# The first two attention units side by side, the second in lent buffers

## The reference

```python
def _attn_ref(q, k, v, alpha):              # (4, 8, 768, 48)
    for t in range(S):
        state = alpha[:, :, t, :, None] * state + einsum('bhd,bhe->bhde', k[:, :, t], v[:, :, t])
        y[:, :, t] = einsum('bhd,bhde->bhe', q[:, :, t], state)

def _moe_ref(x, domain_probs, w1, w2):      # x (3072, 384), 4 experts of 1024
    p = domain_probs / (domain_probs.sum(-1, keepdims=True) + 1e-09)
    for e in range(E):
        out += p[:, e:e + 1] * (maximum(x @ w1[e], 0.0) @ w2[e])

def _moe2_ref(x, w_in, w_out):              # 384 -> 2048 -> 384
    h = x @ w_in
    return (h - tanh(h)) @ w_out
```

## Time and profile before

| what | us |
|---|---|
| median of 3 runs | 1432.39 (1431.64 to 1432.49) |
| the profiled execution, its own time | 1432.69 |
| span of its records | 1430.4 |
| first matmul of unit 0 / of unit 1 / of the dense work | 14.35 / 51.39 / 101.30 |
| PE busy | 1353.6 (95% of the span) |
| DVE / ACT / POOL busy | 864.1 / 559.9 / 296.9 |
| mean granted clock of TensorE | 0.977 of full speed |

### The profile page before, as it was taken

How to read it: one execution, slowest core, us unless ns; L and a number is a source line. 1 busy time by engine, 2 the same in 40 slices (tenths; PEclk the granted TensorE clock), 3 DMA queues, 4 the chain that set the end, 5 groups by cost and what they waited for, 6 DMA issues and landing times.

```text
span 1430.4 us, 25628 instructions
## 1 busy us (share of the span) xinstructions
PE 1353.6 (95%) x10177; PEld 1134.4 (79%) x10177; DVE 864.1 (60%) x1660; ACT 559.9 (39%) x1004; POOL 296.9 (21%) x292
## 2 busy tenths in 40 slices
PE   3438999999999999999999999999999999999999
PEld 2436878898888898787888787889887889888888
DVE  7647484698464487455487546478646458433386
ACT  1222424683223474221375131376131356311175
POOL 5555665400403000312200131300131000000000
PEclk9669999999999999999999999999999999999999
DMA  6228769686655664655565655565555465555552
GB/s 179 73 85 303 263 232 332 234 310 219 218 193 192 223 214 166 220 198 190 195 235 187 208 193 195 185 240 193 191 204 186 155 214 197 187 210 198 177 199 88
DMA packets 104965, 289.05 MB, mean 202 GB/s; under 512 B 10032, under 2 KB 64912, under 8 KB 104848
## 3 DMA queue, kind: packets, MB, share of 16 engines
q1 hardware_dynamic: 104848, 287.43, 58.6%
HBM read 242.52 MB, written 42.52 MB: 199 GB/s over the span
## 4 chain that ended last, share of the span: by engine, by line
PE 87%; DVE 7%; issue 3%; ACT 1%; DMA 0%; SPq 0%; POOL 0%; DVEq 0%; ACTq 0%
PE bank L567 14%; PE bank L568 13%; PE bank L569 13%; PE bank L590 9%; PE bank L591 9%; PE bank L592 9%; PE bank L615 4%; PE bank L613 4%; PE bank L614 4%; PE bank L488 4%; PE bank L523 2%; PE bank L510 1%; DVE R L867 1%; PE bank L466 1%; PE bank L499 1%
## 5 line engine op out<-in xcount | busy, mean ns | idle before, releaser
L743 ACT ACTIVATE HH<-GG 128x512 fp32r<-128x512 f32 x192 | 121.2, 631 | 666.6 <-PE bank L592 532.4
L567 PE MATMUL bank<-XB,RG 128*128 128x512 f32 x864 | 350.3, 405 | 7.1 <-DMA XB<-XS 6.8
L568 PE MATMUL bank<-XB,RG 128*128 128x512 f32 x864 | 340.6, 394 | 0.0
L569 PE MATMUL bank<-XB,RG 128*128 128x512 f32 x864 | 339.6, 393 | 0.0
L941 DVE SCALAR_TENSOR_TENSOR GG<-bank,PB 128x512 f32<-128x512 f32 x192 | 133.2, 694 | 337.6 <-PE bank L569 337.4
L590 PE MATMUL bank<-HH,RG 128*128 128x512 f32 x576 | 224.7, 390 | 1.5 <-ACT OUT L776 1.5
L1080 POOL TENSOR_TENSOR KU<-KU,TOT 128x256 f32<-128x256 f32 x96 | 75.5, 814 | 717.3 <-PE bank L488 717.3
L591 PE MATMUL bank<-HH,RG 128*128 128x512 f32 x576 | 224.3, 389 | 0.0
L592 PE MATMUL bank<-HL,RG 128*128 128x512 f32 x576 | 224.2, 389 | 0.0
L567 PEld LDWEIGHTS bank<-XB,RG 128*128 128x128 f32 x864 | 163.0, 189 | 48.1 <-issue 7.1
L569 PEld LDWEIGHTS bank<-XB,RG 128*128 128x128 f32 x864 | 163.0, 189 | 35.8
(11 more groups left out here) (77 smaller groups left out, 1672.8 us busy)
## 6 DMA issues: line engine op xcount, KB each, us to landing
RG<-scratch SPq DMA_DIRECT2D x240, 768.0 KB, 4.3
scratch<-RG SPq DMA_DIRECT2D x48, 768.0 KB, 5.2
VS<-vp SPq DMA_DIRECT2D x12, 768.0 KB, 6.1
AU<-qka SPq DMA_DIRECT2D x12, 512.0 KB, 5.3
R<-qka SPq DMA_DIRECT2D x12, 512.0 KB, 5.3
KU<-qka SPq DMA_DIRECT2D x12, 512.0 KB, 5.9
WS<-w SPq DMA_DIRECT2D x32, 192.0 KB, 3.0
PB<-probs SPq DMA_DIRECT2D x6, 1024.0 KB, 7.4
```

The source lines that it names most:

```text
L567: nc.tensor.matmul(out, w1(g, 0, kt), x_part(m, 0, kt), start=(kt == 0), stop=False)
L568: nc.tensor.matmul(out, w1(g, 0, kt), x_part(m, 1, kt), start=False, stop=False)
L569: last = nc.tensor.matmul(out, w1(g, 1, kt), x_part(m, 0, kt), start=False, stop=(kt == KT - 1))
```

## The change

Unit 1 gets tiles of its own, which lie over tiles of the dense layers that nothing uses before the dense work (`lend`: KU over SQ, AU over TH, R0, R1 and R2 over HH, HL and GG, SC over QD, QB over LG, KJ and the tables over XB1, VS over OUT), and semaphores of its own. All later units use the old tiles; unit 2 follows unit 0 in them. Units 0 and 1 have four banks each. For every engine the order of the two units' steps is written out. The decay tables of unit 0 and the spreading of the first two units' queries go from POOL to DVE, which starts with them; the probabilities go to the middle of DVE's order, their transpose behind both units' `turn`. POOL makes unit 1's tables between its key steps, waits for `rotated[1]` before it splits the first four weight slots, and then prepares unit 2. `attend` makes the half with the features that have to be moved first, `high_x` and `low_x` copy those first, and `move` starts its first two DMAs when they are there. `join` no longer begins with the copy that needs the last `rotate`. Left out below are the renamed semaphores and tiles of functions that are otherwise the same, and `stated`, `faded` and `carried` counted by set.

```diff
-RING_ALONE = 6
+RING_ALONE = 4
...
+def own(u):
+
+    return int(u == 1)
...
+        def lend(name, words, owner, room, skip=0):
+
+            assert skip + words <= room, name
+            return nc.alloc_sbuf_tensor_at(name, [P, words], fp32, offset=offset[owner] + 4 * skip)
...
+        KU = [place("KU", UW), lend("KUb", UW, "SQ", 2 * TB)]
+        AU = [place("AU", UW), lend("AUb", UW, "TH", 2 * TB)]
+        R0 = [place("R0", QL), lend("R0b", QL, "HH", 4 * TB)]
+        R1 = [place("R1", QL), lend("R1b", QL, "HL", 4 * TB)]
+        R2 = [place("R2", QL), lend("R2b", QL, "GG", 4 * TB)]
+        SC = [place("SC", UW), lend("SCb", UW, "QD", 2 * TB)]
+        QB = [place("QB", UW), lend("QBb", UW, "LG", 2 * TB)]
+        KJ = [place("KJ", UW), lend("KJb", UW, "XB1", 2 * KT * TB)]
+        VS = [place("VS", CHUNKS * VW), lend("VSb", CHUNKS * VW, "OUT", TT * DM)]
...
+        TOT = [place("TOT", TOTALS), lend("TOTb", TOTALS, "XB1", 2 * KT * TB, UW)]
...
-            n = u * FILLS + k
-            return bank[2 + n % RING_ALONE] if u < AHEAD else a_bank[n % 2]
+            return bank[RING_ALONE * u + k % RING_ALONE] if u < AHEAD else a_bank[k % 2]
...
             def move(u):
-                sp.wait_ge(x_low, 3 * u + 3)
-                for hh in range(2):
-                    for j in range(KT):
+                for j in (2, 0, 1):
+                    sp.wait_ge(x_low[own(u)], 3 * turn_of(u) + (2 if j == 2 else 3))
+                    for hh in range(2):
                         src = XS[CH * hh + SPARE * j:CH * hh + SPARE * (j + 1), :].rearrange("p (h t) -> p h t", h=2)
                         dst = x_tile(u)[CH * hh + D:CH * hh + CH, :, j, x_tokens(u)]
-                        sp.dma_start(dst.bitcast(fp32), src.bitcast(fp32)).then_inc(moved, 16)
+                        sp.dma_start(dst.bitcast(fp32), src.bitcast(fp32)).then_inc(moved[own(u)], 16)
...
+            for u in range(AHEAD):
+                load(AU[u][:, :], u, 2, a_in[u])
+                load(R1[u][:, 0:UW], u, 0, q_in[u])
+                load(KU[u][:, :], u, 1, k_in[u])
+                if u == 0:
+                    sp.dma_start(masks[:, :], mask_d).then_inc(masks_in, 16)
+            sp.dma_start(ident[:, :], ident_d).then_inc(ident_in, 16)
+            sp.dma_start(prob[:, :], dp_d).then_inc(prob_in, 16)
+            for u in range(AHEAD):
+                load_values(u)
             for g in range(STAGES):
                 stage(g)
-            for t in range(STAGGER + STEPS):
-                if t < STEPS:
-                    attention(0, t)
-                if t >= STAGGER:
-                    attention(1, t - STAGGER)
-                if t == 2:
-                    sp.wait_ge(prob_laid, 1)
-                    sp.dma_start(probs_d, PT[0:E * NTB * TT, :]).then_inc(prob_saved, 16)
-                    sp.wait_ge(prob_saved, 16)
-                    probs(0)
+            attention(0, 4)
+            attention(0, 7)
+            attention(0, 11)
+            sp.wait_ge(prob_laid, 1)
+            sp.dma_start(probs_d, PT[0:E * NTB * TT, :]).then_inc(prob_saved, 16)
+            sp.wait_ge(prob_saved, 16)
+            probs(0)
+            attention(0, 15)
+            move(0)
+            move(1)
...
-                    c = n * 2 * UC + m
+                    c = (1 - n) * 2 * UC + m
...
-            pe.wait_ge(const_in, 48)
+            diagonal(0)
+            scores(0, 0, 0)
+            diagonal(1)
+            scores(0, 0, 1)
+            scores(1, 0, 0)
+            scores(0, 1, 0)
+            scores(1, 0, 1)
+            scores(0, 1, 1)
+            scores(0, 2, 0)
+            scores(0, 2, 1)
+            scores(1, 1, 0)
+            turn(0, 0)
+            turn(0, 1)
+            scores(1, 1, 1)
+            deltas(0, 0)
+            deltas(0, 1)
+            scores(1, 2, 0)
+            scores(1, 2, 1)
+            turn(1, 0)
+            turn(1, 1)
             pe.wait_ge(prob_step, E + 2)
-            nc.tensor.transpose(h_bank[0][0:E * NTB * TT, 0:P], prob[:, :], ident[:, :]).then_inc(prob_turned, 1)
-            for t in range(STAGGER + STEPS):
-                if t < STEPS:
-                    attention(0, t)
-                if t >= STAGGER:
-                    attention(1, t - STAGGER)
+            nc.tensor.transpose(bank[3][0:E * NTB * TT, 0:P], prob[:, :], ident[:, :]).then_inc(prob_turned, 1)
+            attend(0, 0)
             pe.wait_ge(prob_laid, 1)
+            attend(0, 1)
+            deltas(1, 0)
+            deltas(1, 1)
+            attend(1, 0)
+            attend(1, 1)
...
-                nc.scalar.activation(x[:, 0, 0:2, t], fill_bank(u, 18)[:, :].rearrange("p (a t) -> p a t", a=2),
-                                     ACT.Copy).then_inc(x_high, 1)
-                act.wait_ge(filled, filled_at(u, 19))
-                nc.scalar.activation(x[:, 0, 2, t], fill_bank(u, 19)[:, 0:UT], ACT.Copy).then_inc(x_high, 1)
+                act.wait_ge(filled[own(u)], filled_at(u, 18))
                 if u:
-                    act.wait_ge(moved, 96 * u)
-                nc.scalar.activation(XS[:, 0:UT], fill_bank(u, 19)[:, UT:2 * UT], ACT.Copy).then_inc(x_high, 1)
+                    act.wait_ge(moved[own(u - 1)], 96 * turn_of(u - 1) + 96)
+                nc.scalar.activation(XS[:, 0:UT], fill_bank(u, 18)[:, UT:2 * UT], ACT.Copy).then_inc(x_high[own(u)], 1)
+                nc.scalar.activation(x[:, 0, 2, t], fill_bank(u, 18)[:, 0:UT], ACT.Copy).then_inc(x_high[own(u)], 1)
+                act.wait_ge(filled[own(u)], filled_at(u, 19))
+                nc.scalar.activation(x[:, 0, 0:2, t], fill_bank(u, 19)[:, :].rearrange("p (a t) -> p a t", a=2),
+                                     ACT.Copy).then_inc(x_high[own(u)], 1)
...
-            split = 0
-            for t in range(STAGGER + STEPS):
-                if t < STEPS:
-                    attention(0, t)
-                if t >= STAGGER:
-                    attention(1, t - STAGGER)
-                if t == 0:
-                    act.wait_ge(prob_turned, 1)
-                    nc.scalar.activation(PT[0:E * NTB * TT, :], h_bank[0][0:E * NTB * TT, 0:P],
-                                         ACT.Copy).then_inc(prob_laid, 1)
-                if t in (3, 4, 5, 6):
-                    split_high(t - 3)
+            for g in range(LEAD):
+                split_high(g)
+            lay(0, 0)
+            lay(0, 1)
+            join(0)
+            act.wait_ge(prob_turned, 1)
+            nc.scalar.activation(PT[0:E * NTB * TT, :], bank[3][0:E * NTB * TT, 0:P], ACT.Copy).then_inc(prob_laid, 1)
+            carry(0)
+            lay(1, 0)
+            lay(1, 1)
+            join(1)
+            high_x(0)
+            carry(1)
+            high_x(1)
...
             def low_x(u):
                 x, t = x_tile(u), x_tokens(u)
-                dve.wait_ge(x_high, 3 * u + 1)
-                nc.vector.tensor_tensor(x[:, 1, 0:2, t], fill_bank(u, 18)[:, :].rearrange("p (a t) -> p a t", a=2),
-                                        x[:, 0, 0:2, t].bitcast(fp32), ALU.subtract).then_inc(x_low, 1)
-                dve.wait_ge(x_high, 3 * u + 3)
-                nc.vector.tensor_tensor(x[:, 1, 2, t], fill_bank(u, 19)[:, 0:UT], x[:, 0, 2, t].bitcast(fp32),
-                                        ALU.subtract).then_inc(x_low, 1)
-                nc.vector.tensor_tensor(XS[:, UT:2 * UT], fill_bank(u, 19)[:, UT:2 * UT], XS[:, 0:UT].bitcast(fp32),
-                                        ALU.subtract).then_inc(x_low, 1)
+                dve.wait_ge(x_high[own(u)], 3 * turn_of(u) + 2)
+                nc.vector.tensor_tensor(XS[:, UT:2 * UT], fill_bank(u, 18)[:, UT:2 * UT], XS[:, 0:UT].bitcast(fp32),
+                                        ALU.subtract).then_inc(x_low[own(u)], 1)
+                nc.vector.tensor_tensor(x[:, 1, 2, t], fill_bank(u, 18)[:, 0:UT], x[:, 0, 2, t].bitcast(fp32),
+                                        ALU.subtract).then_inc(x_low[own(u)], 1)
+                dve.wait_ge(x_high[own(u)], 3 * turn_of(u) + 3)
+                nc.vector.tensor_tensor(x[:, 1, 0:2, t], fill_bank(u, 19)[:, :].rearrange("p (a t) -> p a t", a=2),
+                                        x[:, 0, 0:2, t].bitcast(fp32), ALU.subtract).then_inc(x_low[own(u)], 1)
...
+            def tabulate(u, first=0, last=9):
+                n = 9 * turn_of(u)
+                for i in range(first, last):
+                    t, two, three = tables(u, i // 3)
+                    if i:
+                        dve.wait_ge(tabled[own(u)], n + i)
+                    if i % 3 == 0:
+                        out, a, b = two, t[:, :, 0:3], t[:, :, 1:4]
+                    elif i % 3 == 1:
+                        out, a, b = three, two[:, :, 0:2], t[:, :, 2:4]
+                    else:
+                        out, a, b = total(u, i // 3 + 1).rearrange("p (n a) -> p n a", a=1), three[:, :, 0:1], t[:, :, 3:4]
```

(137 more changed lines are left out.)

394 lines of the change are left out of this document (168 added, 226 removed).

## The result

| | before | after |
|---|---|---|
| median | 1432.02 us (4 runs) | 1415.3 us (4 runs, 1413.88 to 1416.52) |
| profiled execution | 1432.69 us, span 1430.4 | 1413.88 us, span 1412.0 |
| first dense matmul | 101.30 | 84.59 |
| from there to the end of the span | 1329.1 | 1327.4 |

The ratio is 0.9881, 95% interval 0.9869 to 0.9894: 1.2% faster, 16.7 us by the medians where 10.2 were forecast. The profiled execution is the fastest of the four, so its 18.4 us of span overstate the typical gain a little.

The account below looks back on a forecast made before the run. PE bounds the dense work, so only its start counts, set by DVE work and hand-overs: 5.5 + 45.2 + 14.4 = 65.1 for the last pick, tail to 91.1, 10.2 us earlier than 101.3; 1432.39 - 10.2 = 1422.2 us, range 1411 to 1428.5.

Parts of the forecast that it names:

- The dense work untouched: After the first dense matmul: the change touches none of these matmuls; only their start moves, 10.2 us earlier.
- half the waits: Case in the front with half of DVE's waits gone: dense start near 82.5, time 1413.5 us.
- Turns: DVE and POOL instructions on SBUF exclude each other: 18 DVE waits, 13.7 us, before unit 1's last pick.
- 45.2 of work: DVE's summed work up to unit 1's last pick, tables through probabilities, at prices from the profile, without waits.
- The walk: Both engines' orders stepped in time with turns on SBUF: last pick at 65.1, dense start at 91.1, ±3.
- The tail: From pick(1,2,0) at 62.6 through attend(0), states(1) to 78.3 and both units' moves: dense start at 91.1.
- The rest: Dense start to end of span: lasts as before, 1329.1 us, ±2.5.
- No turns, or half: Rival in the front: without turns dense start 73.9, 1405.0 us; half 82.5, 1413.5; chance 0.14 for a start before 85.
- The hand-over eats the gain: Rival in the tail: one XS makes the units run one after the other; start 101 to 103, about 1432; chance 0.06.
- Unfair turns: Rival in the front: DVE waits for two POOL instructions each time; doubled, start 111, 1442 us; chance 0.04.
- The clock: Rival at the dense start: clock loss after PE's longer idle doubles, adding 5.5 us, 1428; chance 0.08.
- PE's two waits for join and lay: Before the change, two pieces called "issue", 6.84 and 11.29 us, in which PE waits for ACT.

Follow-up runs that it names:

- its variant: Kernel before with only POOL's four weight splits moved from step 10 of unit 1 to behind prepare(2); 1427.56 us, ratio 0.9965.
- units in turn: Changed kernel with only the order put back: each engine does all of unit 0, then all of unit 1; 1419.97 us, ratio 0.9911.
- tables on POOL: Changed kernel with unit 0's nine tables back on POOL instead of DVE; 1415.63 us.
- two XS: Changed kernel with a second XS tile for unit 1, lent by weight slot RG7, so high_x(1) need not wait for move(0); 1412.82 us.
- transpose early: Changed kernel with the probabilities' transpose ahead of turn(1) in PE's order instead of behind it; 1412.72 us.
- the last kernel: Changed kernel with two XS, POOL held until states(1) ends, transpose early, unit 1's moves on two queues, and the longer hold; 1406.53 us, ratio 0.982.
- the fifth split held: Changed kernel in which POOL waits for unit 2's first rotate before splitting the fifth weight slot; 1414.79 us.
- the longer hold: Changed kernel with POOL's fifth weight split held until queries_up[0] reaches 3 (unit 2's level-1 queries complete); 1415.98 us.

## Why the prediction held, point by point

- *The dense work untouched, the gain all in front of it.* Right: 16.7 of the span's 18.4 us are the earlier start.
- *The number.* In range, but with luck. The start was forecast at 91.1, between 86 and 96 with a chance of 0.68, and came at 84.59. The forecast's own range of time began at 1417; 1415.3 is inside the stated one only because that had been reached down to half the waits, for safety. Of the 6.5 us by which the start was forecast too late, some 5.5 are turns, net of errors of price, and 0.9 is DVE's start (5.5 taken, 4.62 measured).
- *Turns.* Right as a mechanism, by the ends of the instructions in the kernel before. Mis-sized as a term: this is the step behind most of the error. I had 18 waits of 13.7 us before the last pick. DVE is busy from 4.62 to 58.70, 54.1 us; less my own 45.2 of work and 0.7 of gaps, 8.2 are left for turns and errors of price. One such error goes the other way: unit 0's nine tables, priced 2.9, took 4.0 with POOL idle. The walk put keys(1,1) beside rotate(1,1), 5.0 us with 2.1 of waits; in the trace POOL was waiting for PE then, and the rotate took 2.27. It put 1.5 into the tables, where POOL had not yet got its decays, and 0.6 into states(0); both had none. Rotate(0,1) and spread_distant(1), 3.9 of work and 5.7 of waits by the walk, took 7.8. Against that, distant of unit 0 and rotate(0,2) met turns that I did not have, 1.3 and 0.9.
- *The tail.* Every link came as laid out: attend(0) behind turn(1), the transpose, PT and carry(0), 61.25 (66.8 taken); states(1) to 70.9 (78.3), first issue 71.6 (79.1), high_x(1) at the landing of move(0), 77.85 (84.3), PE's pause 9.8 us (9.5). Two errors partly cancel in it: from attend(0) to the end of states(1) 9.7 us for 11.5 taken, and from the first issue to the dense start 13.0 us for 12.0, where one of the issues took 1.41 us in place of 0.63.
- *The rest.* Taken as equal, measured 1.7 us shorter. The stretch of 30 us from the dense start, in the trace of before and of after:

```profile
101.30:131.30 30.00, 26.19 (x264) 20.20 (x264) 22.97 (x43) 7.43 (x12) 12.45 (x8) 0.83 0.82 282
```

```profile
84.59:114.59 30.00, 26.18 (x269) 20.24 (x270) 24.18 (x44) 8.20 (x12) 12.89 (x9) 0.88 0.85 285
```

 Columns: stretch, length, busy us of PE, weight loads, DVE, ACT and POOL, then the granted clock, the share of the DMA engines and GB/s. PE is busy as long, at a clock of 0.88 instead of 0.83, so more is done. The difference lies behind PE's pause of 3.8 us: over the 5 us from 15 us after the dense start on, the clock is 0.77 instead of 0.50. The six kernels with 0.83 or 0.84 over the 30 us (before, its variant, units in turn, tables on POOL, two XS, transpose early) have rests of 1328.7 to 1329.2, the seven with 0.86 to 0.88 of 1327.4 to 1327.9; the last kernel, with a longer pause, has 0.82 and 1329.8. The clock thus accounts for about 1.5 of the 1.7 us (0.05 of 30 us); what decides when it rises after PE's pause was not tried.
- *Rivals.* "No turns, or half" came close: the start of 84.6 is inside its band of below 85, with turns of 8 us in place of 13.7. Not because an instruction is not in the way, but because fewer meet. "The hand-over eats the gain" names real waits, of which the early transpose took out 2.0 us and the second XS 3.3 behind the states; they did not eat the gain. Unfair turns: in the rows read, no single wait on DVE was longer than one POOL instruction. The clock: the loss after the pause did not double, the rest was 1.7 us shorter.
- *Missed altogether.* I took the side-by-side order for the source of the gain. It is worth 4.7 us of the 16.7; the rest of the change with the units in turn already gives 12. The prediction named PE's two waits for join and lay as part of a unit's latency, but gave the new order of ACT no price of its own; by the traces it took some 6 us out.

## What to carry to other kernels

Write out where two engines that share a port meet before writing an order: a POOL instruction of 1.9 us beside a dependent row of short DVE instructions costs one POOL instruction for each, and moving it by three steps was worth 4.4 us in the kernel before. Then ask whether the row is on the path at all: with ACT laying the keys before join, the same rotate could take 4.36 us and cost nothing. A wait like that can only be moved to where DVE is off the path; if DVE is busy up to the next thing that PE needs, the turn comes back under another name. And when two pieces of work are interleaved, look at what single tile is still shared between them: one staging tile put 3.3 us of serial transfers back.

## What had not been expected of the hardware

- Identical code takes its turns differently from one execution to the next. The fade at 66 us took 0.42 us in the changed kernel, where it stood ahead of POOL's next instruction (66.03 against 66.20), and with the same program up to there 2.30 in the kernel with the fifth split held, where it came behind it (66.94 against 66.68):

```profile
66.94 2.30 DVE L965 TENSOR_TENSOR ST<-ST,T 112x192 f32<-112x192 f32 x1
```

 The dense start of these two, and of the one with the longer hold, came at 84.59, 85.69 and 86.54. An effect of less than 2 us in the start of one execution is not to be read without looking at the links.
- Which engine goes first can hang on a third. The three L936 at 17.71 took 1.87 us in the changed kernel, and in the one with the longer hold

```profile
17.78 3.67 DVE L936 TENSOR_TENSOR R<-R,TOT 128x256 f32<-128x256 f32 x3
```

 In both, POOL's key multiplication starts 0.13 us after PE's scores end, at 18.32 and at 17.72. In the first, two of the three L936 have had their turn by then, at 0.42 each, and only the third waits (1.20); in the second POOL is ahead of all three. The 32 score matmuls took 1.56 us in the one and 0.89 in the other, at a granted clock recorded as 1.00 in both; why is open.
